# A gated-attention and mixture-of-experts kernel: phase sums evacuated one slot later, router weights loaded per expert, more warming products before the first slot

## The reference

```
# 1. linear attention, B=4, H=8, S=768, D=48
for t in range(S):
    state = alpha[:, :, t, :, None] * state + k_t (outer) v_t
    y[:, :, t] = q_t @ state
x = y.transpose(0, 2, 1, 3).reshape(3072, 384)
# 2. four experts, all used for every token, F=1024
p = domain_probs / (domain_probs.sum(-1, keepdims=True) + 1e-9)
x = sum over e of p[:, e:e+1] * (relu(x @ w1[e]) @ w2[e])
# 3. gated feed-forward, d_ff=2048
h = x @ w_in
out = (h * clip(h + 3, 0, 6) / 6) @ w_out
```

## Time and profile before

| | us |
|---|---|
| median of 3 runs (lowest to highest) | 1417.92 (1414.83 to 1418.27) |
| profiled execution, its own time | 1416.81 |
| its span in the trace | 1415.0 |
| TensorE busy in the span | 1377.4 |
| VectorE, ScalarE, GpSimd busy | 731.7, 530.5, 796.6 |

### The profile page before, as it was taken

The page is one execution under the profiler, slowest core; times in us unless marked ns, Lnnn a source line. Parts: engine busy times, 40 slices in busy tenths (PEclk is TensorE's granted clock), DMA queues, the critical chain, the costliest instruction groups (busy, mean ns, idle before and its releaser), DMA issues.

```text
span 1415.0 us, 31885 instructions
## 1 busy us (share of the span) xinstructions
PE 1377.4 (97%) x12464; PEld 1118.9 (79%) x12464; DVE 731.7 (52%) x1401; ACT 530.5 (37%) x992; POOL 796.6 (56%) x860
## 2 busy tenths in 40 slices
PE   7799999999999999999999999999999999999998
PEld 5578888788888788888788888878888888888887
DVE  8766664545554555555555555455555433333333
ACT  2233333333354333344333335433335433335443
POOL 7866665655655565656565656556555344444442
PEclk9899999999999999999999999999999999999999
DMA  4443333333334333334343333433332433333341
GB/s 143 132 122 108 104 107 96 96 113 101 101 99 144 109 106 95 109 100 136 88 121 116 96 104 102 136 115 103 97 93 82 120 112 101 98 93 94 97 123 34
DMA packets 70371, 150.20 MB, mean 106 GB/s; under 512 B 9296, under 2 KB 21840, under 8 KB 70224
## 3 DMA queue, kind: packets, MB, share of 16 engines
q1 hardware_dynamic: 70224, 148.16, 35.6%
HBM read 143.36 MB, written 4.77 MB: 105 GB/s over the span
## 4 chain that ended last, share of the span: by engine, by line
PE 94%; issue 1%; DVE 0%; DVEq 0%
PE h_bank L468 42%; PE out_banks L484 29%; PE out_third L484 14%; PE score_banks L394 4%; PE score_banks L432 1%; PE score_banks L440 1%; PE state_bank L415 1%; PE state_bank L405 1%; PE h_bank L448 0%; DVE p_kept L576 0%; DVE result L635 0%; PE out_banks L432 0%; PE out_banks L440 0%; DVEq L138 0%; DVE p_kept L565 0%
## 5 line engine op out<-in xcount | busy, mean ns | idle before, releaser
L857 POOL TENSOR_TENSOR w_lo<-w_raw,w_hi 128x768 fp32r<-128x768 f32 x288 | 531.3, 1845 | 565.2 <-ACT w_hi L760 564.5
L754 ACT ACTIVATE h_hi<-h_bank 128x512 fp32r<-128x512 f32 x288 | 172.5, 599 | 667.0 <-DVE h_bank L609 589.1
L468 PE MATMUL h_bank<-x_hi,w_hi 128*128 128x512 f32 x864 | 338.9, 392 | 12.0 <-issue 12.0
L468 PE MATMUL h_bank<-x_hi,w_lo 128*128 128x512 f32 x864 | 338.1, 391 | 0.0
L468 PE MATMUL h_bank<-x_lo,w_hi 128*128 128x512 f32 x864 | 338.1, 391 | 0.0
L609 DVE SCALAR_TENSOR_TENSOR h_bank<-h_bank,probs 128x512 f32<-128x512 f32 x192 | 134.1, 698 | 324.6 <-PE h_bank L468 324.6
L760 ACT ACTIVATE w_hi<-w_raw 128x768 fp32r<-128x768 f32 x288 | 241.3, 838 | 0.0
L484 PE MATMUL out_banks<-h_hi,w_hi 128*128 128x512 f32 x576 | 232.8, 404 | 0.0
L484 PE MATMUL out_banks<-h_hi,w_lo 128*128 128x512 f32 x576 | 225.2, 391 | 0.0
L484 PE MATMUL out_banks<-h_lo,w_hi 128*128 128x512 f32 x576 | 225.2, 391 | 0.0
L621 DVE TENSOR_TENSOR h_lo<-h_bank,h_hi 128x512 fp32r<-128x512 f32 x288 | 197.0, 684 | 48.0 <-ACT h_hi L754 48.0
(11 more groups left out here) (76 smaller groups left out, 1207.5 us busy)
## 6 DMA issues: line engine op xcount, KB each, us to landing
w_raw<-w SPq DMA_DIRECT2D x288, 384.0 KB, 3.1
alpha_q<-qa SPq DMA_DIRECT2D x48, 256.0 KB, 3.6
k_raw<-kk SPq DMA_DIRECT2D x48, 128.0 KB, 3.5
probs<-prob_scratch SPq DMA_DIRECT2D x6, 1024.0 KB, 8.0
v_diag<-v SPq DMA_DIRECT2D x96, 48.0 KB, 2.4
out<-result SPq DMA_DIRECT2D x18, 256.0 KB, 3.9
level_sb<-level SPq DMA_DIRECT2D x1, 80.0 KB, 3.2
ident_sb<-ident SPq DMA_DIRECT2D x1, 64.0 KB, 2.9
```

The source lines that it names most:

```text
L468: mm = pe.matmul(h_bank[g % 2][:, :], a, x, start=k == 0 and i == 0, stop=k == K3 - 1 and i == 2)
L754: act.activation(h_hi[:, g % DEEP, :], h_bank[g % 2][:, :], ACT.Copy).then_inc(hh_made, 1)
L857: pool.tensor_tensor(w_lo[:, g % RING, :], w_raw[:, g % RAW, :], w_hi[:, g % RING, :].bitcast(F32), ALU.subtract).then_inc(w_lo_made, 1)
```

## The change

Four edits. (1) `collect` on VectorE and `x2_hi` on ScalarE stand one slot later: in slot S + 2, `collect` after `hidden_lo(S + 1)`. (2) ScalarE's `split_x` stands before `weights_hi` in its slot instead of last. (3) `load_probs` takes one expert (256 KB in place of 1024 KB) and has a semaphore of its own for each; in the prologue only expert 0 of tile 0 is loaded, the other 23 loads each stand in SyncE's slot E_START[t] + 8 (e - 1), that is eight slots before use. (4) In the prologue's last chunk `keep_warm` gets 5 products before `attend` instead of 1, and 4 after it instead of 1 and 1.

```
+PROBS_AT = {max(E_START[t] + FT * (e - 1), 0): (t, e) for t in range(TILES) for e in range(EXPERTS) if t + e}
-        in_p = [sem(f"in_p{i}") for i in range(2)]
+        in_p = [[sem(f"in_p{i}_{e}") for e in range(EXPERTS)] for i in range(2)]
# sync
-            def load_probs(t):
+            def load_probs(t, e):
                 if t >= 2:
-                    sp.wait_ge(h_out, E_START[t - 2] + E_SLOTS)
-                sp.dma_start(probs[:, t % 2, :, :], prob_scratch[:, t * TILE:(t + 1) * TILE].rearrange(
-                    "(o e) n -> o e n", o=1).to_broadcast([P, EXPERTS, TILE])).then_inc(in_p[t % 2], 16)
+                    sp.wait_ge(h_out, E_START[t - 2] + (e + 1) * FT)
+                sp.dma_start(probs[:, t % 2, e, :], prob_scratch[e:e + 1, t * TILE:(t + 1) * TILE].to_broadcast([P, TILE])
+                             ).then_inc(in_p[t % 2][e], 16)
...
-                    load_probs(0)
-                    load_probs(1)
+                    load_probs(0, 0)
...
-                for t in range(2, TILES):
-                    if g == E_START[t] - 8:
-                        load_probs(t)
+                if g in PROBS_AT:
+                    load_probs(*PROBS_AT[g])
# tensor
-                keep_warm(1)
+                keep_warm(1 if n + 1 < PER_TILE else 5)
                 attend(n)
-                keep_warm(1)
+                keep_warm(1 if n + 1 < PER_TILE else 4)
                 if n + 1 < PER_TILE:
                     turn_k(n + 1)
-                keep_warm(1)
+                    keep_warm(1)
# vector
-                dve.wait_ge(in_p[t % 2], 16 * (t // 2 + 1))
+                dve.wait_ge(in_p[t % 2][u], 16 * (t // 2 + 1))
...
-                if g >= BEHIND and g - BEHIND + 1 in STARTS:
-                    collect(PHASE_OF[g - BEHIND])
+                if g > BEHIND and g - BEHIND in STARTS:
+                    collect(PHASE_OF[g - BEHIND - 1])
# scalar
-                if g >= BEHIND and g - BEHIND + 1 in STARTS and PHASES[PHASE_OF[g - BEHIND]][0] == "E":
-                    x2_hi(PHASE_OF[g - BEHIND])
+                if g > BEHIND and g - BEHIND in STARTS and PHASES[PHASE_OF[g - BEHIND - 1]][0] == "E":
+                    x2_hi(PHASE_OF[g - BEHIND - 1])
                 if PHASES[PHASE_OF[g]][0] == "M":
                     gate_hidden(g)
                 hidden_hi(g)
+                if g in STATE_AT:
+                    split_x(STATE_AT[g])
                 if g + SPLIT_AHEAD < SLOTS:
                     weights_hi(g + SPLIT_AHEAD)
...
-                if g in STATE_AT:
-                    split_x(STATE_AT[g])
```

## The result

| | us |
|---|---|
| before, median of 4 runs (lowest to highest) | 1417.34 (1414.83 to 1418.27) |
| changed kernel, median of 4 runs | 1396.92 (1395.96 to 1397.57) |
| ratio, 95% interval | 0.9858 (0.9841 to 0.9875) |
| profiled execution of the changed kernel: own time, span | 1396.57, 1394.7 |

The change makes the kernel 20.4 us faster by the medians, 20.2 us between the two profiled executions. The forecast was 1395.7, a gain of 21.1.

A forecast was written before the change was run, and what follows sets the result against it. TensorE, busy 1377.4 of 1415.0 us, was taken as the bound, so time could come only from its waits and slow stretches: 12.0 + 5.4 + 2.0 + 1.7 = 21.1 us off 1416.81, giving 1395.7 us, range 1392.5 to 1401.0.

The forecast's parts named there:

- The waits: Ends of phases: TensorE's five waits at `hidden` vanish once `hidden_lo(S + 1)` no longer waits for `collect`, -12.0 us.
- The slow slots behind them: Slots behind four of the waits at `hidden`: return to 4.08 us when the waits go, -5.4 us.
- (c): Rival: sums 0.6 us late at four ends with attention work, clock falling after each, 9.3 us, 1405.0; chance 0.04.
- The residual: Ends with attention work: `project(S)` might wait for late sums; 0 taken, at most 4 x 0.6 = 2.4 us.
- E5's end: End of a late phase, before slot 258: wait of 0.6 us and slow slot of 0.12 us forecast to go.
- Router weights: Prologue: smaller broadcasts shrink TensorE's 3.34 us stop at 57.33 to 1.5 us or less; -2.0 us, bounds 0 and 3.24.
- rival (a): Prologue: the stop is not caused by the broadcasts, so the 2.0 us are not won, 1397.7; chance 0.11.
- Warming: Prologue's last chunk and slot 0: more products keep TensorE at full clock, -1.7 us; other bound +2.5 us.
- The signs: Trace evidence of error: `project(S)` waiting for L632 or L636, clock dip after slot 32, slot 0 not 3 us earlier.
- Rival (d): Slower: VectorE reaches `collect` late at all eleven ends, each followed by a slow slot, costing 25.4 us; chance 0.03.
- two prologue terms: Before and in slot 0: router weights, -2.0 us, and warming, -1.7 us.
- slot terms: Ends of phases: waits at `hidden`, -12.0 us, and the slow slots behind them, -5.4 us.

The follow-up runs named there:

- edit 1 alone: Kernel before with only the sums (`collect`, `x2_hi`) one slot later, ScalarE's `split_x` left last: 1401.44 us, ratio 0.9892.
- edit 3 alone: Kernel before with only the router weights loaded per expert: 1415.14 us over 12 executions, ratio 0.9991 (0.9980 to 1.0002).
- edit 4 alone: Kernel before with only the new warming products in the prologue's last chunk: 1416.79 us over 12 executions, ratio 0.9998 (0.9986 to 1.0009).

## Why the prediction was right or wrong

**The waits (-12.0): right.** None is left at `hidden`, and edit 1 alone shows that the moved `collect` by itself removes them.

**The slow slots behind them (-5.4): right in sum, and more by luck than the working says.** The pair gave the forecast (13.67 us for three ends, 13.23 predicted). But I read the slow slots of one execution as belonging to the M ends and argued in (c) that "even the 3.37 us wait was not followed by a slow slot". With edit 3 alone and with edit 4 alone just that one was (5.79 us). The term should have been a number of slow slots (three in two of these traces, four in the third) at 1.6 to 1.7 us each, not a place for each.

**The residual (0): nearly right.** The four ends with attention work cost nothing, for the reason given: with `split_x` moved the scaling starts before `weights_lo`. Without it they cost 1.5 us (0.24 to 0.73 each, 0.6 forecast), without the slow slots that (c) added. What I missed is E5's end, where no attention work stands in the way: slot 258 takes 0.42 us more than 4.08, since ScalarE's rounding stands behind `weights_hi` and meets the bank 0.6 us late. I had counted VectorE's queue for `collect` and not ScalarE's.

**Router weights (-2.0): not seen in the pair, near in size by the medians, wrong in its mechanism.** Undone it costs 1.8 us, alone it brings 2.2; neither difference is clear of its interval, so 2 us is likely and not shown. And "if the stop at 57.33 shrinks to 1.5 us or less" failed: it stays, at 3.4 us. It is a block border of TensorE's program; at most the broadcasts lengthen it. The one trace that I had held a short stop (3.3) of a kind that took 5.6 to 6.1 in the three other traces with the same broadcasts. So rival (a) describes the pair. That the edit works through a stop that is typically 5.6 us before and 3.4 us after is an inference from one trace to a kernel.

The page that I cited against the term, "Runtime: NRT & Kernel Launch" of the Trainium skill (instruction fetch mechanics), has engines fetch their program in blocks of 256 instructions, at a cost mostly hidden. The stops stand some 256 instructions apart, which agrees. "Mostly hidden" holds at the other borders of the changed kernel's prologue, where TensorE does not stop; at this one the stops are 2.3 to 6.1 us.

**Warming (-1.7): right in the pair, not confirmed by the medians.** `carry(7)` starts alike in both traces and slot 0 ends 1.9 us earlier (0.74 + 1.15), by nearly the steps as forecast. But edit 4 alone brings 0.6 us by the medians and undoing it costs 0.0, and neither interval excludes 1.7. What is unsure is the price of the cold slot 0: I took 3.51 us, from one execution, for what `hidden(0)` costs without warming. In the five traces with the old warming products slot 0 took 4.64 to 5.60 us, with the new ones 4.07 to 4.09: that part is worth 0.6 to 1.5 us, depending on the execution.

**The signs.** One named for a wrong forecast appeared: slot 0 starts 0.74 us earlier and not "some 3". (The forecast's own terms give 2.4, since 1.36 us of the warming lies inside slot 0.) A second appeared in small, the wait of 0.2 us for L632. No dip of the clock was left after slot 32.

**Rival (d)** asked for 25.4 us over eleven ends. Late at all eleven, with `collect` behind the weighing, was 17.3 us: even this form did not reach it. **The sum and the range.** The two prologue terms erred together by 1.7 us in the pair, the slot terms by 0.8 the other way, so the forecast came closer (21.1 us for 20.2) than its terms did, which is luck. The range (1392.5 to 1401.0) was wide enough for either error.

## What to carry to other kernels

Work that an engine does for a buffer due in half a slot should not stand in its queue ahead of work due sooner: write down for each step what it waits for and when its reader needs it, and place the evacuation just behind the step that is due before it. Count this queue by queue, on the engine that rounds as well as on the one that subtracts. Before one trace's slow stretch or stop is booked as a term, see in a second execution that it is at the same place and of the same length.

## What the runs showed of the hardware

- In the prologue, in a stream of 64-row products, TensorE stood for 2.3 to 6.1 us in the middle of a burst that waits for nothing, in eleven traces behind the same instruction of its program. The next program block was being fetched then, and TensorE went on 1.3 to 1.6 us after it had landed. The fetch started 4.0 to 7.6 us after TensorE had entered the block before. With six more products ahead it started 1.1 us after, and the stop was gone; stops of 0.58 to 1.5 us stood at earlier borders.
- A wait in the dense stream is no sure sign of a low clock. Waits of 0.93 and 1.57 us were followed by slots of 4.17 to 4.21 us; waits of 2.2 to 3.4 us were followed by the lower of the two clocks in some traces (window at 0.50, that is 1.2 GHz) and not in others, at 1.6 to 1.7 us a time.
- VectorE's q scaling (128x256, two SBUF inputs) took 0.41 or 0.42 us when it began before GpSimd's subtraction and 1.56 to 1.60 us when the subtraction had begun before it. The order of two short instructions on ScalarE, 0.33 and 0.84 us, decides which.
